# Attention, spectral mixing and two MLPs on one core: masks and dots turned one step later, channel tables loaded behind a fold, a shorter row lag

## The reference

```python
q_assign = argmax(q_n @ c_n.T); k_assign = argmax(k_n @ c_n.T)      # nearest centroid of each row
scores = where(q_assign[:, None] == k_assign[None, :], q @ k.T / 8, -1e9)
x = softmax(scores) @ v                                             # heads side by side: (2, 768, 512)
u = x + real(fft(fft(x, axis=1), axis=2)); un = layernorm(u)
y = u + relu(un @ w_ch1) @ w_ch2                                    # 512 -> 2048 -> 512
h = relu(y @ w_in); gate = sigmoid(conv3_along_tokens(h))           # 512 -> 1024
out = (h * gate) @ w_out                                            # 1024 -> 512
```

## Time and profile before

| what | value |
|---|---|
| time, median of 3 runs | 696.37 us (693.69 to 698.76) |
| the profiled execution | 693.69 us, span 691.5 us |
| PE busy, share of the span | 680.4 us, 98% |
| DVE, ACT, POOL busy | 48%, 39%, 34% |
| granted TensorE clock, mean | 0.995 |

### The profile page before, as it was taken

The page is one execution under the profiler, slowest core; times in us unless marked ns, Lnnn a source line. Parts: engine busy times, 40 slices in busy tenths (PEclk is TensorE's granted clock), DMA queues, the critical chain, the costliest instruction groups (busy, mean ns, idle before and its releaser), DMA issues.

```text
span 691.5 us, 9621 instructions
## 1 busy us (share of the span) xinstructions
PE 680.4 (98%) x3666; PEld 551.2 (80%) x3666; DVE 332.8 (48%) x598; ACT 272.7 (39%) x522; POOL 232.2 (34%) x252
## 2 busy tenths in 40 slices
PE   8899999999999999999999999999999999999998
PEld 7676676767777689888888888888888899988886
DVE  4786776777766629743114211141111489944300
ACT  4765666666666622211112111121111377744411
POOL 5745878649585050678400000000150060000000
PEclk8999999999999999999999999999999999999999
DMA  5453436424453201233100000010140620000111
GB/s 172 143 134 98 125 99 154 113 74 110 132 137 111 70 1 31 77 107 107 46 1 0 1 1 0 1 61 1 31 153 1 182 62 1 1 31 16 46 47 46
DMA packets 26493, 47.03 MB, mean 68 GB/s; under 512 B 3792, under 2 KB 10832, under 8 KB 26448
## 3 DMA queue, kind: packets, MB, share of 16 engines
q1 hardware_dynamic: 23392, 38.08, 19.7%
q0 software_dynamic: 2912, 7.95, 3.8%
q10 hardware_dynamic: 144, 0.39, 0.2%
HBM read 35.98 MB, written 3.15 MB: 57 GB/s over the span
## 4 chain that ended last, share of the span: by engine, by line
PE 93%; DVE 5%; ACT 1%; issue 1%; POOL 0%; DVEq 0%; POOLq 0%
PE ps L1586 19%; PE ps L1552 19%; PE ps L1347 10%; PE ps L1648 10%; PE ps L1333 9%; PE ps L1634 9%; PE ps L1322 6%; PE ps L1323 5%; PE ps L1431 1%; PE ps L1401 1%; PE ps L1356 1%; PE ps L1486 1%; PE ps L1277 1%; PE ps L1294 0%; DVE xt_l L1207 0%
## 5 line engine op out<-in xcount | busy, mean ns | idle before, releaser
L1155 DVE SCALAR_TENSOR_TENSOR hid_l<-ps,hid_h 128x512 fp32r<-128x512 f32 x48 | 33.2, 692 | 196.1 <-ACT hid_h L801 196.1
L907 DVE TENSOR_REDUCE row_min<-ps 128x1 f32<-128x768 f32 x96 | 91.8, 957 | 62.0 <-PE ps L1323 61.1
L801 ACT ACTIVATE hid_h<-ps 128x512 fp32r<-128x512 f32 x48 | 28.7, 598 | 223.7 <-PE ps L1552 223.7
L687 ACT ACTIVATE prob<-ps,row_min 128x768 f32<-128x768 f32 x96 | 86.6, 902 | 14.0 <-DVE row_min L907 13.0
L1333 PE MATMUL ps<-cst,prob 128*128 128x128 f32 x576 | 81.7, 274 | 1.0 <-DVE pt L915 0.6
L1322 PE MATMUL ps<-k,q 80*128 80x384 f32 x192 | 74.4, 387 | 2.3 <-ACT prob L687 1.4
L1586 PE MATMUL ps<-w_h,hid_h 128*128 128x512 f32 x192 | 76.2, 397 | 0.0
L1586 PE MATMUL ps<-w_h,hid_l 128*128 128x512 f32 x192 | 75.5, 393 | 0.0
L1333 PEld LDWEIGHTS ps<-cst,prob 128*128 128x128 f32 x576 | 68.3, 141 | 8.2 <-issue 1.9
L1586 PE MATMUL ps<-w_l,hid_h 128*128 128x512 f32 x192 | 74.7, 389 | 0.0
L1347 PE MATMUL ps<-pt,v_n 128*64 128x384 f32 x384 | 72.1, 498 | 0.3 <-DVE x L991 0.3
(11 more groups left out here) (175 smaller groups left out, 1370.2 us busy)
## 6 DMA issues: line engine op xcount, KB each, us to landing
w_raw<-in_moe_w_ch SPq DMA_DIRECT2D x24, 256.0 KB, 2.5
raw_d<-in_q SPq DMA_DIRECT2D x8, 384.0 KB, 3.5
v_n<-in_v SPq DMA_DIRECT2D x16, 192.0 KB, 2.6
out<-out_s SPq DMA_DIRECT2D x12, 256.0 KB, 2.0
raw_qk<-in_k SPq DMA_DIRECT2D x15, 192.0 KB, 3.2
raw_qk<-in_q SPq DMA_DIRECT2D x15, 192.0 KB, 3.7
q<-q SPq DMA_DIRECT2D x15, 192.0 KB, 3.3
k<-k SPq DMA_DIRECT2D x15, 192.0 KB, 3.6
```

The source lines that it names most:

```text
L687: nc.scalar.activation(prob[t % 2][:, :, :].rearrange("p (h j) c -> p h (j c)", h=2), ps[:, 2 * (t % 2):2 * (t % 2) + 2, 0:HALF], ACT.Exp, ...
L907: nc.vector.tensor_reduce(row_min[:, col:col + 1], ps[:, 2 * (t % 2):2 * (t % 2) + 2, 0:HALF], axis=AX.XY, op=ALU.min).then_inc(min_ready, 1)
```

## The change

Four edits.

1. In attention the dots, their transposes and the mask's transposes move. On PE the dots stand behind step 0 of the next head and both kinds of transposes behind its step 1, in every head (head 0 had the dots' part so already). ACT and DVE are reordered to fit: `store_dots` behind step 0, `store_mask` behind step 1, `masks` behind `store_right(m, 0)`, `largest_dot`, `hits` and `weigh_hits` one place further on each, `first_hit` at the start of the odd head. ACT's last steps are written out, in the order that they had.
2. The sequence tables are loaded in two DMAs (in rounds 12 and 13) instead of six, and PE waits for 32 instead of 96.
3. POOL's wait for the scores of head 14 goes, and `fold_block(0, 3)` stands ahead of the two loads of channel tables.
4. ROW_LAG is 2 instead of 3, on PE and ACT.

```diff
-ROW_LAG = 3
+ROW_LAG = 2
@@ POOL
-                if n in (12, 13, 14):
+                if n in (12, 13):
                     if n == 12:
                         pool.wait_ge(dots_ready, UNITS_M)
-                    r = n - 12
-                    for part, table in enumerate((seq_h, seq_l)):
-                        nc.gpsimd.dma_start(table[:, r, :], seq_tab[:, part, r, :]).then_inc(seq_loaded, 16)
+                    part = n - 12
+                    nc.gpsimd.dma_start((seq_h, seq_l)[part][:, :, :],
+                                        seq_tab[:, part, :, :]).then_inc(seq_loaded, 16)
...
-            pool.wait_ge(score_ready, NT * (NH - 1))
+            fold_block(0, 3)
             nc.gpsimd.dma_start(ch_h[:, :, :], chan_tab[:, 0, :, :]).then_inc(ch_loaded, 16)
             nc.gpsimd.dma_start(ch_l[:, :, :], chan_tab[:, 1, 0:2 * KC, :]).then_inc(ch_loaded, 16)
-            fold_block(0, 3)
             fold_block(1, 3)
@@ ACT head
                 store_left(n, 4)
-                if n and n % 2 == 0 and u < UNITS_M:
-                    store_dots(u)
                 exponent(n + 1, 1 - s, 0)
...
                 step(n + 1, 1 - s, 0)
-                if n == 0:
+                if n % 2 == 0 and u < UNITS_M:
                     store_dots(u)
+                step(n + 1, 1 - s, 1)
                 if n % 2 and u < UNITS_M:
                     store_mask(u)
-                step(n + 1, 1 - s, 1)
-                step(n + 1, 1 - s, 2)
+                exponent(n + 1, 1 - s, 3)
+                store_left(n + 1, 2)
                 step(n + 1, 1 - s, 3)
@@ DVE head
+                if masking:
+                    first_hit(u)
                 step(n, s, 4)
                 denominator(n, s, 0)
-                if n == 1:
-                    first_hit(u)
-                if masking:
-                    masks(u)
+                minimum(m, 1 - s, 1)
                 invert(n, 0)
-                minimum(m, 1 - s, 1)
                 store_right(n, 5)
...
+                invert(n, 1)
                 store_right(m, 0)
-                invert(n, 1)
-                if n and dotting:
-                    largest_dot(u)
-                    hits(u)
+                if masking:
+                    masks(u)
                 minimum(m, 1 - s, 3)
                 store_right(m, 1)
-                if n == 0:
+                if dotting:
                     largest_dot(u)
                 minimum(m, 1 - s, 4)
                 store_right(m, 2)
-                if n == 0:
+                if dotting:
                     hits(u)
-                if n and dotting:
-                    weigh_hits(u)
-                    first_hit(u)
                 step(m, 1 - s, 3)
-                if n == 0:
+                if dotting:
                     weigh_hits(u)
@@ PE head
                 step(n, s, 4)
-                if n and dotting:
-                    dots(u)
                 if n:
                     values(n - 1, VALUES_AT[2][1])
                 step(n, s, 5)
                 if n:
                     fold_o(n - 1)
-                if n and dotting:
-                    turn_dots(u)
-                if masking:
-                    turn_mask(u)
                 step(nxt, 1 - s, 0)
-                if n == 0:
+                if n % 2 == 0 and u < UNITS_M:
                     dots(u)
                 values(n, VALUES_AT[0][1])
                 step(nxt, 1 - s, 1)
-                if n == 0:
+                if n % 2 == 0 and u < UNITS_M:
                     turn_dots(u)
+                if n % 2 and u < UNITS_M:
+                    turn_mask(u)
                 step(nxt, 1 - s, 2)
@@ PE, before the last head
-            pe.wait_ge(seq_loaded, 32 * R)
+            pe.wait_ge(seq_loaded, 32)
```

More of the change, by code:

```diff
@@ L1370, in head @@
                 nxt, u = n + 1, n // 2 + 2
-                dotting, masking = n % 2 == 0 and u < UNITS_M, n % 2 == 1 and u < UNITS_M
                 step(n, s, 4)
-                if n and dotting:
-                    dots(u)
                 if n:
```

## The result

| what | before | after |
|---|---|---|
| median, 4 runs each on one chip | 697.12 us | 706.02 us (703.51 to 706.92) |
| the profiled execution | 693.69 us, span 691.5 us | 703.59 us, span 701.7 us |

The ratio is 1.0129, 95% interval 1.0081 to 1.0177: slower by 1.3%. I had forecast slower by 0.55%, 700.2 us, and 705.0 as the upper end. The sign was right, and the size was less than half of what came. From profiled execution to profiled execution I had +3.8 us, and the span grew by 10.2; from median to median it is 8.9, with an interval of 5.6 to 12.3.

What follows compares the result with a forecast made beforehand. TensorE, busy 98% of the span, was taken as the bound, so only gaps in its stream count. Terms -1.0 + 1.5 + 0 + 2.3 + 1.0 = +3.8 us on the median 696.37 gave 700.2 us, range 695.5 to 705.0.

Steps and rivals of the forecast that it cites:

- Reordering, -1.0: Attention heads 2 to 12: transposes behind step 1 hide behind DVE's copy, 10 steps shorter by 0.1 us, -1.0 us.
- Rival D: Attention: the reordering gains more, transposes vanish in a TensorE wait, 11 x 0.33 = -3.6 us more, 696.6 us; chance 0.10.
- Mask rows later, +1.5: Before heads 5, 9 and 13 TensorE waits 0.6 us each for later mask rows, where 0.34 was waited once: +1.5.
- Sequence tables in two DMAs, 0 to +0.5: POOL's larger table loads share DMA engines with head 14's k load; taken as 0, bounded by +0.5 us.
- Table wait, +2.3: Before the channel products TensorE waits 2.3 us for channel tables issued behind fold_block(0, 3).
- rival B: Channel products: the clock falls to half in the table wait, costing another 3.4 us stretch, 703.6 us; chance 0.10.
- ROW_LAG, +1.0: Tail, narrow of tile 6: the last gated tile's low part is 0.94 us late, +1.0 us with the semaphore.
- Rival A: Heads 5 and 9: mask rows queue behind raw loads, landing 4.2 instead of 1.9 us, +4.6, 704.8 us; chance 0.12.
- Rival C: Whole kernel: table loads are the only wait, mask rows and narrow covered; 694.7 us, or 697.4 on the median; chance 0.13.

Runs made afterwards that it cites:

- M_S_late: Kernel before with edits 1 and 2, the second sequence table issued in round 14 instead of round 13; span 693.4 us.
- D_raw: Kernel before with only dots and their transposes moved, raw q and k loads issued behind mask rows, k and w1 in odd rounds; 693.22 us against 695.45.
- no_C: The changed kernel without edit 3; 702.11 us against 695.83 for the kernel before, ratio 1.0113.
- C_early: Kernel before, POOL waiting for x of head 14 instead of its scores, then loading channel tables, then fold_block(0, 3); span 698.9 us.

## Why the prediction was right or wrong

- *Reordering, -1.0.* Right: -1.1, with 3.01 for 3.11 in eleven steps. One of them I had thought lost in head 3's wait. Rival D, more than 0.1 a head, is out.
- *Mask rows later, +1.5.* This step failed, by +3.5: the waits grew by 5.0. Head 13 makes 2.7 of it (3.27 for 0.6). The times of issue were right: T = 194.10, first issue at T+1.2, the last at T+3.15, TensorE's arrival at T+4.7. Wrong was "lands 1.9 after its issue", a number from a quiet queue at 191.69, used for a DMA that the change itself moves into the microseconds in which POOL issues a table. I had counted what stands in front of it in its queue, and not what another queue would have under way at the new time. `M_S_late`, with no table near, has the landing of 1.9 and a wait of 0.66 again. Of the rest, head 5 has +0.4 (SP's slow issue) and head 9 +0.2, and head 7 has +0.8, against 0.6 less before head 3. These last two are luck of the execution more than the change: the raw loads in front of their rows left 0.63 of slack before head 7 in the trace of before, and kernels with unchanged attention wait there too. I had priced only heads whose mask changes.
- *Sequence tables in two DMAs, 0 to +0.5.* Failed, and it is the same failure from the other side. I wrote that the table shares the DMA engines with the k load of head 14, and left out the 24 KB of mask rows issued 0.12 us ahead of it. Alone the edit costs 0.1, beside edit 1 it costs 2.6 more. Pricing edits one by one could not find it.
- *Table wait, +2.3.* Right: 2.2, and 2.26 alone; landing 4.9 after the issue of ch_l, 5.5 from that of ch_h. By the estimate from the Trainium skill ("DMA: Bandwidth & Descriptors", section "Anatomy of one DMA — SWDGE (gpsimd) path") both tables would have landed 4.7 after the first issue; the measured 5.5 decides. What went with it, the clock behind the wait, stood only in rival B.
- *ROW_LAG, +1.0.* Right in mechanism, mis-sized: 1.4 in after, 1.25 of it at this wait. The low part was ready at 669.52, 11.45 behind the last widen (11.44 forecast); TensorE's matmul for it would have started at 668.41, 10.3 behind it rather than 10.5, and 0.15 went between the release and the second matmul of the tile.
- *Rival A, +4.6 through late landings.* It wasn't this: the last rows of heads 5 and 9 landed 1.9 and 2.1 after issue, as its own "against" said, and their waits stayed near 1. Head 13 got a landing of 4.5, from a table in another queue. Its own mechanism, rows behind raw loads, hit head 7 (4.8).
- *Rival C.* Out: both the mask rows and the narrow waited.
- *Rival B, the clock falls in the table wait.* It happened, at 1.3 and not 3.4, and a second time behind head 13. I gave it 0.10, though the trace of before had no idle time of this length once the clock was up. That was no evidence for the forecast's side: a wait longer than any in the trace should have carried its clock cost in the upper end of the range.

In numbers: +3.8 forecast and +10.2 found differ, in these two executions, by 3.5 (mask rows and table), 2.9 (clock, twice), 0.4 (tail), -0.1 (table wait) and -0.3 (shorter steps).

## What to carry to other kernels

When an edit moves a small DMA that somebody waits for, list everything that all queues have under way at its new time, with sizes, and price its landing from a row of the trace that has such company; and price edits that move DMAs and edits that enlarge them as a pair. A wait of TensorE can cost more than itself: behind each one of 2.2 us or more in these traces the clock fell, so carry that in the range. And put large loads with slack behind the small ones that are due, as `D_raw` does; it cost nothing here. Before giving the place of a wait to an edit, see whether kernels without that edit have it too.

## What the runs showed of the hardware

- A DMA of 24 KB landed 1.9 us after its issue alone, 3.4 when one of 385 KB was issued 0.1 us behind it from another engine's queue (and a second 0.6 later), and 4.5 when that had 1155 KB (4.4 in `no_C`). Being first by 0.1 us didn't protect it. In its own queue, 4 to 5 us behind loads of 384 KB, the last of four took 3.7 to 5.9 in the kernel before and up to 6.4 in `C_early`; in `D_raw`, with these loads behind it, 1.9.
- The granted clock fell from 2.4 to 1.2 GHz behind idle times of the weight loader of 2.17, 2.25, 3.10 and 3.23 us, and in one of 8.84, each time after 58 to 246 us at 2.4 GHz with TensorE nearly always busy; it didn't behind 1.42 (in the tail), 1.56 (by the length of the steps) and 2.11. A stretch at 1.2 GHz was 3.4 us long and cost 1.3 to 1.6, that of the longest idle time 10.2 us long and cost 2.2.
- SP's slow issues (over 0.9 us instead of 0.4 to 0.6) came nearly always, 46 of 48 times, beside a 16 KB transfer in the queue called "instruction". That these make them isn't shown. That the falls of the clock follow from the idle time alone wasn't tested apart from what TensorE did before.
